# Counting one more slot in the rules for transfers and weight jobs of an attention and feed-forward kernel

## The reference

```python
# 2 batches, 8 heads, 768 positions, head size 64; 4 sink keys, window of 128
scores = scale * q @ k.T                      # kept: own last 128 keys and the 4 sinks
a = exp(scores - max); a = a / (sum(a) + 1e-9)
x = (a @ v), heads side by side               # 1536 tokens x 512
y = (silu(x @ w_gate) * (x @ w_val)) @ w_out  # "B", 512 -> 1536 -> 512
h = y @ w_in
out = (max(h, 0) + alpha * min(h, 0)) @ w_out2  # "C", 512 -> 2048 -> 512
```

## Time and profile before

| what | us |
|---|---|
| median of 3 runs | 651.46 (651.22 to 655.24) |
| the profiled execution, its own time | 656.12 |
| its span, first to last instruction | 654.4 |
| around the span | 1.72 |
| PE busy | 632.8 |
| POOL busy | 451.3 |
| mean granted TensorE clock | 0.984 of full speed |

### The profile page before, as it was taken

The page is one execution under the profiler, slowest core; times in us unless marked ns, Lnnn a source line. Parts: engine busy times, 40 slices in busy tenths (PEclk is TensorE's granted clock), DMA queues, the critical chain, the costliest instruction groups (busy, mean ns, idle before and its releaser), DMA issues.

```text
span 654.4 us, 9479 instructions
## 1 busy us (share of the span) xinstructions
PE 632.8 (97%) x3111; PEld 494.6 (76%) x3111; DVE 405.0 (62%) x689; ACT 246.2 (38%) x597; POOL 451.3 (69%) x597
## 2 busy tenths in 40 slices
PE   8997977998999999999999999999999999999998
PEld 5565755775777788888888888888888888888886
DVE  5844353553548795647475656599775677656474
ACT  5744425352544553213021212245543244433150
POOL 6965564767687889989899945679999987820000
PEclk9998989997999999999999999999999999999999
DMA  9074134231122301212122223010222222000005
GB/s 303 17 210 114 40 107 146 64 98 51 50 84 65 94 18 53 77 32 65 34 65 82 65 65 98 16 49 17 65 66 64 66 65 82 16 1 1 0 6 189
DMA packets 34016, 45.69 MB, mean 70 GB/s; under 512 B 2888, under 2 KB 15176, under 8 KB 33968
## 3 DMA queue, kind: packets, MB, share of 16 engines
q1 hardware_dynamic: 33824, 44.83, 22.5%
q10 hardware_dynamic: 144, 0.26, 0.2%
HBM read 41.93 MB, written 3.15 MB: 69 GB/s over the span
## 4 chain that ended last, share of the span: by engine, by line
PE 89%; DMA 5%; POOL 2%; ACT 2%; DVE 1%; issue 1%; SPq 0%; DVEq 0%; POOLq 0%; ACTq 0%
PE ffn_ps L2051 27%; PE att_ps L2026 23%; PE ffn_ps L1936 14%; PE att_ps L2051 7%; PE ffn_ps L2026 6%; DMA raw_weights<-pieces 4%; PE att_ps L1890 3%; PE att_ps L1847 2%; PE att_ps L1865 2%; POOL w_lo L1705 1%; PE att_ps L1936 1%; ACT scratch L2108 1%; POOL w_hi L1704 1%; DMA k_sb<-kt 1%; PE ffn_ps L1847 0%
## 5 line engine op out<-in xcount | busy, mean ns | idle before, releaser
L1705 POOL TENSOR_TENSOR w_lo<-raw_weights,w_hi 128x512 fp32r<-128x512 f32 (+1 forms) x128 | 154.2, 1204 | 10.3
L1704 POOL CAST w_hi<-raw_weights 128x512 fp32r<-128x512 f32 (+1 forms) x128 | 78.9, 617 | 62.0 <-DMA raw_weights<-pieces 35.8
L2413 DVE TENSOR_TENSOR scratch<-ffn_ps,scratch 128x512 f32<-128x512 f32 x108 | 74.0, 686 | 35.7 <-PE ffn_ps L2051 35.1
L1733 POOL TENSOR_TENSOR w_lo<-part_sum,w_hi 128x256 fp32r<-128x256 f32 x80 | 60.9, 762 | 6.4
L1936 PE MATMUL ffn_ps<-x_hi,w_hi 128*128 128x512 f32 x152 | 64.5, 424 | 0.1
L1936 PE MATMUL ffn_ps<-x_hi,w_lo 128*128 128x512 f32 x152 | 61.7, 406 | 0.0
L1936 PE MATMUL ffn_ps<-x_lo,w_hi 128*128 128x512 f32 x152 | 61.6, 406 | 0.0
L2051 PE MATMUL ffn_ps<-h_hi,w_hi 128*128 128x512 f32 x130 | 52.6, 404 | 0.0
L2051 PE MATMUL ffn_ps<-h_lo,w_hi 128*128 128x512 f32 x130 | 51.3, 394 | 0.0
L2051 PE MATMUL ffn_ps<-h_hi,w_lo 128*128 128x512 f32 x130 | 51.2, 394 | 0.0
L1786 POOL TENSOR_TENSOR scratch<-scratch,inv 128x264 f32<-128x264 f32 (+1 forms) x48 | 30.7, 639 | 26.2 <-DVE inv L2290 26.0
(11 more groups left out here) (211 smaller groups left out, 1585.6 us busy)
## 6 DMA issues: line engine op xcount, KB each, us to landing
raw_weights<-pieces SPq DMA_DIRECT2D x122, 256.0 KB, 2.8
k_sb<-kt SPq DMA_DIRECT2D x12, 264.0 KB, 3.6
v_sb<-vt SPq DMA_DIRECT2D x12, 256.0 KB, 3.5
out<-scratch SPq DMA_DIRECT2D x12, 256.0 KB, 2.0
q_sb<-qt SPq DMA_DIRECT2D x11, 256.0 KB, 4.3
scratch<-vs SPq DMA_DIRECT2D x1, 384.0 KB, 7.6
q_sb<-qt ACTq DMA_DIRECT2D x1, 256.0 KB, 3.6
scratch<-vs SPq DMA_DIRECT2D x1, 16.0 KB
```

Of the source, the lines that this page charges most:

```text
L1704: chain(pool.tensor_copy(hi, raw[:, r % n_raw, at]))
L1705: last = pool.tensor_tensor(lo, raw[:, r % n_raw, at], hi.bitcast(F32), ALU.subtract)
L1733: pool.tensor_tensor(lo, s, hi.bitcast(F32), ALU.subtract).then_inc(split_done, 1)
L2413: ins = dve.tensor_tensor(to, back_ps(key), total, ALU.add)
```

## The change

Three numbers move by one. In the deal of weight jobs, even slots get one job and odd slots two (before: the other way round); slots with a `tsum` still get one. In SP's loop, values of quad c come in step 4c-4 instead of 4c-5, and keys of quad c+1 in the step after that, n with n % 4 equal to 1, instead of n % 4 equal to 0.

```diff
-        for _ in range(1 if n % 2 or plan[slot_plan[n] + 1][0] == "tsum" else 2):
+        for _ in range(1 if n % 2 == 0 or plan[slot_plan[n] + 1][0] == "tsum" else 2):
...
-                if n_pairs * c - 5 <= n and c < n_quads:
+                if n_pairs * c - 4 <= n and c < n_quads:
                     load_values(c)
                     c += 1
-                if n_pairs * c - 8 <= n and n % n_pairs == 0 and c < n_quads and c > RING + 1:
+                if n_pairs * c - 7 <= n and n % n_pairs == 1 and c < n_quads and c > RING + 1:
                     load_keys(c)
```

## The result

| | us |
|---|---|
| before, median of its runs beside this one | 653.35 (651.22 to 656.49, 4 runs) |
| after, median | 633.01 (632.92 to 633.26, 4 runs) |
| ratio | 0.9686, 95% interval 0.9637 to 0.9734 |
| forecast | 631.5 (627 to 640) |

The profiled execution of the changed kernel took 633.01 us with a span of 631.3, the one before 656.12 with 654.4. The difference of the two is 23.1 us; the prediction's sum said 22.4.

The account below looks back on a forecast made before the run. PE was taken to be bound by four stalls behind POOL's normalise, worth 22.4 us. 656.12 - 22.4 = 633.7 and 651.46 - 22.4 = 629.1; the middle, 631.5 us, was forecast, range 627 to 640.

Parts of the forecast that it names:

- What bounds the kernel: Between 42 and 229 us, four PE transposes wait 14.2 us for POOL's normalise, behind weight pieces held by keys gates.
- Price of the stalls: Slots 24, 28, 32 and 40 against stall-free slot lengths: 22.4 us, 14.2 idle and 8.2 slow.
- The deal of jobs: From slot 20 on, odd slots get two weight jobs; claimed to cost POOL and PE nothing.
- part 1: The change's new deal of weight jobs: no job moves by more than one slot, at no cost.
- part 2: The change's new SP order: first piece behind a keys gate delays a normalise needed one slot later, so no stall.
- The walk behind a gate: From gate slot's start S: split starts at S + 6.88 (slot 27) or 6.48 (slot 35), leaving 0.9 us or more spare.
- Rivals A: At the keys gates, one or two smaller stalls remain, at most 5 us each: 636.5 us, chance 0.08.
- D: Two jobs in the gate's slot put POOL behind, four stalls costing 7.5 us each: 659 us, chance 0.03.
- rival C: At the keys gates, each stall stays but shifts one slot on: 651 us, chance 0.04.
- Rival B: After 229 us, POOL's late jobs don't move up with PE, losing 6.8 us: 638 us, chance 0.05.
- The predicted median: Whole kernel: 631.5 us, the middle between 629.1 (difference common to before and after) and 633.7 (stalls and clock hit one execution).
- What the profile would show: Between 42 and 210 us, normalise waits gone or under 2 us; stalled slots at clock 1.00; chain transfers 2% or less.

Follow-up runs that it names:

- e4: Kernel before with only the values' transfers one step later in SP's loop; keys and deal of jobs unchanged: 654.12 us, ratio 0.9989.
- e3: Kernel before with only the keys' transfers one step later in SP's loop; values and deal of jobs unchanged: 635.2 us, ratio 0.9683.
- e6: Kernel before with values and keys one step later, except one quad's keys (slot 27's gate) left at the old step: 638.29 us, ratio 0.9737.
- e2: Kernel before with only the deal of weight jobs moved, SP's order unchanged: 645.71 us, ratio 0.9858.
- e1: Kernel before with only SP's order moved, values and keys one step later, deal of jobs unchanged: 633.24 us, ratio 0.9657.
- e5: Kernel before plus products nobody reads, ahead of the four stalled transposes to keep PE busy: 647.17 us, ratio 0.9867.

## Why the prediction was right

- *What bounds the kernel.* Right: four stalls of PE's transposes, behind normalise, behind the split of a piece that a keys gate holds back. e4 leaves them all, e3 removes them, e6 brings one back.
- *Price of the stalls.* 22.4 us from the lengths of the slots; the same slots measured 22.66 less. The 0.3 between is in the yardsticks: slots 24, 28 and 32 without a stall took 5.73, 5.49 and 5.48, for 5.81, 5.59 and 5.59 in the sum. The estimate that went by the Trainium skill (TensorE: Matmul & The Clock Gate, "HAM oscillation"), 24.4, was further off than the rows' 22.4 against the 23.1 of the whole difference: half of the throttled time is lost only where PE has products in it. In e2, where nearly all of it had, half the throttled time closed the sum to 0.2 us.
- *The deal of jobs.* Priced at nothing and, beside SP's order, measured at nothing (e1 against the whole change). But the prediction argued part 1 and part 2 as one pattern, in which the first piece behind K8 has to be a job of slot 27. They are two cures for the same stall: each removes the old four (e1, e2), and only the one in SP's order brings no new ones. So the deal wasn't needed, and by itself it is worth 1.4%, not nothing.
- *The walk behind a gate.* Split start at S + 6.88 and 6.48: measured S + 6.17 in slot 27 (78.62 - 72.45) and 6.23 in slot 35. The spare time at K8 was 1.8 by the walk and 2.05 in the trace, at K10 0.9 and 1.16. Rivals A and D, which lived on this margin, did not come about, and rival C fell with it. That rests on four executions of the whole change, of which one has a profile.
- *Given back later.* Rival B did not come: from 229 us on PE waited for nothing before the change, and waits for nothing now, and the saving arrives whole at the end. Its argument had a wrong reading, that POOL is busy almost all the time after 229 us. There POOL is busy for 293.0 of 425.4 us (0.69), and of its 33 us of waits there nearly 30 are for PE, so it moves up with PE.
- *The predicted median.* 631.5 was 1.5 low, and the step that made it so was taking the middle between two readings of the 4.7 us by which the profiled execution lay above the median. One reading was right: the difference lies in how hard the stalls and the clock hit one execution, so that the stall-free time is the profiled execution's, less its stalls: 633.7 by the sum, 633.01 measured. e6 shows it, and so do the 20 runs of the kernel before in the experiments: the three at a mean clock of 0.992 took 651.05 to 651.94, the six at 0.986 to 0.990 took 652.95 to 655.60, the eleven at 0.982 to 0.984 took 654.49 to 658.19, while all runs of kernels without a stall lie between 632.6 and 633.6. The stalls' own length varies too, by less: 14.2 us together in one profile, 14.3 in e4's, about 15 in e5's. That the forecast came within 1.5 us is in part luck: by the other reading alone it would have been 629.1.
- *What the profile would show.* No wait for normalise, slots of 5.8, 5.6, 5.6 and 4.4 (5.73, 5.49, 5.48, 4.37), clock 1.00, transfers at 1% of the chain: all seen. POOL's remaining three waits for pieces are behind K7, K8 and K10, as expected for slots 27 and 35.

## What to carry to other kernels

Where one queue carries urgent and patient transfers in one written order, look for a transfer that waits for the consumer's progress (a gate) and count, for each piece behind it, the slot in which its user stands ahead of something urgent: here a piece due a slot before the gate's cost a stall of 1.9 to 4.1 us, one piece of the gate's own slot cost nothing, and two of them cost between nothing and 1.3 us (0.35 and 0.80 in e3, 1.30 in slot 37 of e2). Such a count, done on the order written out, gave the place of every stall of over 0.4 us in seven variants, and their sizes to about half a microsecond. Price a stall by the length of its whole slot and not by the idle time alone, and when a kernel's runs spread while a stall-free one's would not, take the stall-free time from one execution instead of shifting the median.

## What the runs showed that I had not expected

- The same stall does not always bring the clock down, nor does a longer one bring it down for longer. In the kernel before, slot 28 with 4.12 us of idle time had 3.4 us at half speed, and slot 40 with 3.01 had 6.8. With one stall of 3.7 us in the profile, four runs had mean clocks of 1.000, 0.997, 0.997 and 0.994 (e6); within one execution 2.73 us of idle time left the clock at 2.4 GHz, and 1.90 and 2.27 brought it to 1.2 (e2). So the length of the idle time alone doesn't tell. What else does wasn't tried.
- Products that nobody reads hold the clock well: with them in place of idle time all four runs had 1.00 (e5), worth 4 to 11 us in this kernel. They are a fair second best where a wait can't be removed, and a way to split a stall's price, as long as they are no longer than the wait: beyond it they add their own time.
